# Attention, gated unit and convolution unit on one core: residual added within PSUM, key exponentials behind the x evictions, first output products in pieces

## What is computed

```python
q_s = exp(q - max(q, -1));  q_s = q_s / (sum(q_s, -1) + 1e-9)      # over 64 channels of a head
k_s = exp(k - max(k, 2));   k_s = k_s / (sum(k_s, 2) + 1e-9)       # over the 576 tokens
kv = einsum('bhsd,bhse->bhde', k_s, v)
x = einsum('bhsd,bhde->bhse', q_s, kv)       # (8, 576, 512) after reordering
# first unit
h = gelu_tanh(x @ w_in)                      # 1024 wide: u, v = halves of 512
v_n = layer_norm(v) * g_ln
v_s = einsum('ts,bsd->btd', w_sg, v_n) + b_sg
x1 = x + (u * v_s) @ w_out                   # the residual
# second unit
h = relu(x1 @ w_in2)                         # 1024 wide
c = conv over tokens, 3 taps per channel
y = (h * sigmoid(c)) @ w_out2
```

## Time and profile before

| | us |
|---|---|
| median of 3 runs | 989.21 (989.05 to 991.13) |
| the profiled execution | 990.6 |
| its span, first to last instruction | 988.8 |
| mean granted share of TensorE's clock | 0.988 |

### The profile page before, as it was taken

How to read it: one execution, slowest core, us unless ns; L and a number is a source line. 1 busy time by engine, 2 the same in 40 slices (tenths; PEclk the granted TensorE clock), 3 DMA queues, 4 the chain that set the end, 5 groups by cost and what they waited for, 6 DMA issues and landing times.

```text
span 988.8 us, 15996 instructions
## 1 busy us (share of the span) xinstructions
PE 941.2 (95%) x6652; PEld 909.6 (92%) x6652; DVE 619.8 (63%) x935; ACT 376.7 (38%) x560; POOL 353.1 (36%) x222
## 2 busy tenths in 40 slices
PE   6689899899998998999999998999999999999998
PEld 5589799798897997998998997999999999999998
DVE  6794666656747656667356597676767575757560
ACT  4462442433424424334214344343434343434331
POOL 4642634345436345363303322222222222222230
PEclk8899999999999999999999998999999999999999
DMA  9706115034052151241211421010202011110101
GB/s 312 258 15 193 51 45 176 36 81 167 20 154 92 28 181 49 49 136 35 81 49 43 141 73 61 25 66 19 73 25 74 25 57 41 33 65 13 37 25 48
DMA packets 49911, 77.92 MB, mean 79 GB/s; under 512 B 4272, under 2 KB 22704, under 8 KB 48944
## 3 DMA queue, kind: packets, MB, share of 16 engines
q1 hardware_dynamic: 45232, 67.48, 21.4%
q10 hardware_dynamic: 4608, 9.44, 2.5%
HBM read 56.97 MB, written 18.89 MB: 77 GB/s over the span
## 4 chain that ended last, share of the span: by engine, by line
PE 79%; DVE 9%; issue 5%; ACT 3%; DMA 2%; POOL 1%; ACTq 0%; SPq 0%; POOLq 0%; DVEq 0%
PE psum L417 64%; PE psum L409 6%; PE psum L475 4%; DVE plain_arena L1167 2%; PE psum L451 2%; DVE plain_arena L1164 2%; PE psum L556 2%; PE psum L510 1%; DMA plain_arena<-in_q 1%; ACT split_arena L742 1%; POOL plain_arena L1401 1%; DVE split_arena L1089 1%; ACT plain_arena L769 0%; ACT split_arena L723 0%; POOL split_arena L1395 0%
## 5 line engine op out<-in xcount | busy, mean ns | idle before, releaser
L417 PE MATMUL psum<-split_arena 128*128 128x288 f32 x5568 | 765.9, 298 | 28.3 <-DVE split_arena L1089 16.3
L417 PEld LDWEIGHTS psum<-split_arena 128*128 128x128 f32 x5568 | 750.8, 190 | 36.6 <-DVE split_arena L1089 20.8
L1444 POOL TENSOR_TENSOR plain_arena<-plain_arena 128x576 f32<-128x576 f32 x64 | 107.5, 1680 | 294.7 <-ACT plain_arena L934 294.7
L1307 DVE TENSOR_SCALAR plain_arena<-plain_arena 128x576 f32<-128x576 f32 x64 | 39.8, 622 | 113.8 <-ACT plain_arena L928 113.8
L409 PE MATMUL psum<-split_arena 128*128 128x512 f32 x384 | 96.5, 398 | 4.3 <-DVE plain_arena L1164 2.3
L1312 DVE SCALAR_TENSOR_TENSOR plain_arena<-plain_arena 128x576 f32<-128x576 f32 x64 | 97.0, 1516 | 2.2
L1401 POOL TENSOR_TENSOR plain_arena<-plain_arena 128x576 f32<-128x576 f32 x32 | 47.4, 1482 | 126.8 <-DVE plain_arena L1147 126.8
L409 PEld LDWEIGHTS psum<-split_arena 128*128 128x128 f32 x384 | 70.6, 190 | 20.9 <-DVE plain_arena L1164 4.9
L928 ACT ACTIVATE plain_arena<-psum 128x576 f32<-128x576 f32 x64 | 41.5, 649 | 93.8 <-PE psum L417 59.3
L934 ACT ACTIVATE plain_arena<-plain_arena 128x576 f32<-128x576 f32 x64 | 43.7, 683 | 51.5 <-DVE split_arena L1317 44.7
L1317 DVE TENSOR_TENSOR split_arena<-plain_arena,split_arena 128x576 fp32r<-128x576 f32 x64 | 54.0, 843 | 12.2 <-ACT split_arena L940 11.1
(11 more groups left out here) (79 smaller groups left out, 772.7 us busy)
## 6 DMA issues: line engine op xcount, KB each, us to landing
x_dram<-plain_arena ACTq DMA_DIRECT2D x32, 288.0 KB, 2.1
plain_arena<-x_dram SPq DMA_DIRECT2D x8, 1152.0 KB, 5.5
outT<-plain_arena SPq DMA_DIRECT2D x32, 288.0 KB, 2.1
plain_arena<-in_v SPq DMA_DIRECT2D x32, 256.0 KB, 3.2
plain_arena<-in_kT SPq DMA_DIRECT2D x7, 1152.0 KB, 10.2
plain_arena<-in_k SPq DMA_DIRECT2D x7, 1024.0 KB, 5.7
plain_arena<-in_q SPq DMA_DIRECT2D x7, 1024.0 KB, 5.6
plain_arena<-in_w_in SPq DMA_DIRECT2D x8, 512.0 KB, 5.5
```

What stands on the lines that cost most here:

```text
L417: mm = e.matmul(out[:, h, 0:NH], stat[s], mov[m][:, h * NH:(h + 1) * NH], start=first and n == 0, stop=last and n == 2, skip_group_check=True)
L1444: e.tensor_tensor(gt[:, f % 2, :], gt[:, f % 2, :], hp[:, f % 2, 1:T + 1], ALU.mult).then_inc(hg_full, 1)
```

## The change

- `add_x`: L1164 writes its sum back into the PSUM banks, and the second add reads it there and writes `x1`. All waits of TensorE for `o_half` become waits for `o_add`.
- ScalarE, end of a body: `exp_k(n, 0)` moves behind `hi_x(a, 0)`, `exp_k(n, 1)` behind `hi_x(a, 1)`, `exp_k(n, 2)` behind the last store.
- `kv_piece(b, 0)` waits for `v_tail_sum` in place of `v_gelu`.
- Second half: the first two output tiles of batch 0 are made in pieces, `first_y(f)`, each of the twelve products that need tile f. They stand between the last `h_unit` of batch 0 and around the first of batch 1. ScalarE and VectorE split the x of batch 1 two tiles later, and ScalarE's order of copies follows.

```diff
--- before.py
+++ after.py
@@ -466,11 +466,11 @@
                 else:
                     e.wait_ge(v_in[j % 2], 32 * b + 16 * (j // 2))
                 if j == 0 and not (isinstance(b, int) and b <= 1):
-                    e.wait_ge(o_half, (b - 1) * DT - 1)
+                    e.wait_ge(o_add, (b - 1) * DT - 1)
                 elif j == 0 and b == 1:
                     e.wait_ge(kv_lo, 2)
                 if j == 0 and not first(b):
-                    e.wait_ge(v_gelu, b * NU)
+                    e.wait_ge(v_tail_sum, b)
                 for d in range(DT):
                     mm = e.matmul(kv_sums[:, d // 2, d % 2, 0:VW], kn[:, j, d * P:(d + 1) * P], v_place(b, j)[:, d, :],
                                   start=j == 0 and d % 2 == 0, stop=j == NJ - 1, skip_group_check=True)
@@ -492,11 +492,11 @@
                     e.wait_ge(x_lo, 2)
                 if ds[0] == 0 and not (isinstance(b, int) and b == 0):
                     if u == 0:
-                        e.wait_ge(o_half, b * DT - 3)
+                        e.wait_ge(o_add, b * DT - 3)
                     elif u == 1:
-                        e.wait_ge(o_half, b * DT)
+                        e.wait_ge(o_add, b * DT)
                     else:
-                        e.wait_ge(o_half, b * DT - 1)
+                        e.wait_ge(o_add, b * DT - 1)
                 for d in ds:
                     if u == 0:
                         e.wait_ge(x_lo, b * DT + d + 1)
@@ -574,7 +574,7 @@
                     elif isinstance(b, int) and b == B - 1:
                         e.wait_ge(x_lo, B * DT)
                     else:
-                        e.wait_ge(o_half, b * DT + 2)
+                        e.wait_ge(o_add, b * DT + 2)
                 for f in fs:
                     if d == 0:
                         e.wait_ge(g_lo, b * FT + f + 1)
@@ -654,7 +654,7 @@
 
             def h_unit(b, f):
                 if isinstance(b, int) and b == 0 and f < 2:
-                    e.wait_ge(o_half, B * DT - 3 + f)
+                    e.wait_ge(o_add, B * DT - 3 + f)
                 else:
                     e.wait_ge(h_relu, b * F2T + f - 1)
                 for d in range(DT):
@@ -666,22 +666,25 @@
                                      [x2[h][:, d, :] for h in (0, 1)], d == 0, d == DT - 1)
                 mm.then_inc(h_done, 1)
 
-            def y_unit(b, par, d):
-                if isinstance(b, int) and b == 0:
-                    if d == 0:
+            def y_part(b, par, d, fs):
+                if fs[0] == 0:
+                    if b == 0 and d == 0:
                         e.wait_ge(w2_lo, len(W2))
-                    if d == 0:
-                        e.wait_ge(o_half, B * DT - 1)
-                    elif d == 1:
-                        e.wait_ge(o_half, B * DT)
-                if d >= 2 or not (isinstance(b, int) and b == 0):
-                    e.wait_ge(y_copied, b * DT + d - 1)
-                for f in range(F2T):
+                        e.wait_ge(o_add, B * DT - 1)
+                    elif b == 0 and d == 1:
+                        e.wait_ge(o_add, B * DT)
+                    else:
+                        e.wait_ge(y_copied, b * DT + d - 1)
+                for f in fs:
                     if d == 0:
                         e.wait_ge(hg_lo, b * F2T + f + 1)
                     mm = both_halves(y_sets[d % 2], [w2out[h][:, f, d * P:(d + 1) * P] for h in (0, 1)],
                                      [hg[par][h][:, f, :] for h in (0, 1)], f == 0, f == F2T - 1)
-                mm.then_inc(y_done, 1)
+                if fs[-1] == F2T - 1:
+                    mm.then_inc(y_done, 1)
+
+            def y_unit(b, par, d):
+                y_part(b, par, d, list(range(F2T)))
 
             def step(b, par, last=False):
 
@@ -691,9 +694,27 @@
                         h_unit(b + 1, 2 * d + 1)
                     y_unit(b, par, d)
 
-            for f in range(F2T):
+            def first_y(f):
+                y_part(0, 0, 0, [f])
+                y_part(0, 0, 1, [f])
+
+            for f in range(F2T - 1):
                 h_unit(0, f)
-            step(0, 0)
+                if f >= 4:
+                    first_y(f - 4)
+            h_unit(0, F2T - 1)
+            first_y(3)
+            first_y(4)
+            first_y(5)
+            h_unit(1, 0)
+            for f in range(6, F2T):
+                first_y(f)
+            for f in range(1, 4):
+                h_unit(1, f)
+            y_unit(0, 0, 2)
+            for f in range(4, F2T):
+                h_unit(1, f)
+            y_unit(0, 0, 3)
             step(1, 1)
             for k in range(1, B // 2 - 1):
                 step(2 * k, 0)
@@ -904,12 +925,13 @@
                 for d in range(DT):
                     if a is not None and d >= 2:
                         hi_x(a, d - 2)
+                        if n is not None:
+                            exp_k(n, d - 2)
                     store_x1(m, d)
-                    if n is not None and d >= 1:
-                        exp_k(n, d - 1)
                     if a is None and d == 1:
                         hi_x2(0)
                 if n is not None:
+                    exp_k(n, 2)
                     exp_q(n, 2)
 
             first_attention()
@@ -975,18 +997,21 @@
             e.wait_ge(o_done, B * DT)
             e.wait_ge(o_add, B * DT)
             for f in range(F2T + 2):
-                if f == F2T - 2:
-
-
-                    relu(0, f)
-                    sigmoid(0, f - 1)
+                tile_steps(0, 0, f)
+                if f == F2T - 1:
                     hi_x2(1)
-                    hi_hg(0, 0, f - 2)
-                else:
-                    tile_steps(0, 0, f)
                 if f == 2:
                     hi_w2(len(W2) - 1)
-            step(0, 0)
+            copy_y(0, 0)
+            copy_y(0, 1)
+            for f in range(4):
+                tile_steps(1, 1, f)
+            copy_y(0, 2)
+            for f in range(4, F2T + 2):
+                if f == F2T - 1:
+                    hi_x2(2)
+                tile_steps(1, 1, f)
+            copy_y(0, 3)
             step(1, 1)
             for k in range(1, B // 2 - 1):
                 step(2 * k, 0)
@@ -1160,11 +1185,12 @@
                     e.wait_ge(x1_out[d % 2], b * 32 + 16)
                 elif not (isinstance(b, int) and b == 0):
                     e.wait_ge(x1_out[d % 2], b * 32)
-                place = x1[:, d % 2, :]
-                e.tensor_tensor(place.rearrange("p (a b) -> p a b", a=2), o_set(b, d)[:, :, 0:NH],
-                                f32(xT[0][:, d, :]).rearrange("p (a b) -> p a b", a=2), ALU.add).then_inc(o_half, 1)
+                bank = o_set(b, d)[:, :, 0:NH]
+                e.tensor_tensor(bank, bank, f32(xT[0][:, d, :]).rearrange("p (a b) -> p a b", a=2),
+                                ALU.add).then_inc(o_half, 1)
                 e.wait_ge(o_half, b * DT + d + 1)
-                e.tensor_tensor(place, place, f32(xT[1][:, d, :]), ALU.add).then_inc(o_add, 1)
+                e.tensor_tensor(x1[:, d % 2, :].rearrange("p (a b) -> p a b", a=2), bank,
+                                f32(xT[1][:, d, :]).rearrange("p (a b) -> p a b", a=2), ALU.add).then_inc(o_add, 1)
 
             def lo_x2(b):
                 for d in range(DT):
@@ -1322,7 +1348,7 @@
                 for f in range(F2T + 2):
 
 
-                    if x and f == (F2T - 2 if isinstance(b, int) and b == 0 else F2T - 1):
+                    if x and f == (F2T if b == 0 else F2T - 1):
                         lo_x2(b + 1)
                     if f < F2T:
                         convolve(b, f)
```

## The result

| | us |
|---|---|
| before, on the same chip | 989.13 (988.53 to 991.13, 4 runs) |
| after | 973.24 (972.04 to 973.87, 4 runs) |
| ratio | 0.9834, 95% interval 0.9817 to 0.9852 |
| profiled execution of after | 973.65, its span 971.9 |

The account below looks back on a forecast made before the run. TensorE, busy 941 of 988.8 us, was taken to bound the kernel, so only its idle stretches counted. 14.6 − 0.8 + 2.5 − 0.8 = 15.5 us off gave a median of 973.7, range 969.5 to 979.5.

Parts of the forecast that it names:

- boundaries m = 0 to 5: Between batches, `x_piece(a, 2)` starts at 312.20 instead of 314.63: 2.43 us gained, six times, 14.6 us.
- new wait at m = 6: At the last boundary nothing is gained and TensorE waits for tile 1's second add: 0.8 us lost.
- key product's wait, six times: `kv_piece(a, 0)` waiting for `v_tail_sum` gains 0.42 us for m = 1 to 6: 2.5 us.
- second half: Stops of 4.0 and 1.4 us replace the 4.9 one, and the clock falls again: 0.8 us lost.
- The held add: Tile 1's second residual add at a boundary, 2.17 us beside GpSimd's `sub_k`, takes 0.76 when reading PSUM.
- The rival in which it stays held: The second add takes 2.17 us whether reading PSUM or not: 982.3 us, chance 0.08.
- the slower rival: The add writing into PSUM is itself held by GpSimd's three `sub_k`: 1008.7 us, chance 0.05.
- The new wait: At a boundary TensorE stands 0.72 us before `o_part(m, 3)`, until tile 1's second add frees the bank.
- What is next late: At a boundary `v_part` 1 wants tile 3 at 310.43 and starts at 310.83: fits by 0.4 us.
- the restart after a stop: The first product of TensorE after a stop costs 0.1 us more.
- late pieces: Rival: second-half pieces find their inputs late and cost some 3 us beyond the sum: 976.5 us, chance 0.10.
- the case with the clock at 2.4 GHz: Rival: TensorE's clock doesn't fall in the second half, 2.5 us less: 971.2 us, chance 0.25.

Follow-up runs that it names:

- the first run: The kernel before with only the residual adds going through PSUM and TensorE's waits moved to the second add: 978.40 us, ratio 0.9891.
- the bank exchange: The changed kernel with the two main PSUM bank pairs exchanged between output tiles 0 and 1 of the first unit: 971.39 us, ratio 0.9809.
- the later run without the stop: The changed kernel with the first six pieces waiting for only the first seven weight chunks, the eighth awaited ahead of the seventh piece: 966.58 us, ratio 0.9770.

## Why the prediction was right

The forecast of 973.7 lay 0.5 from the median. In the profile, which the sum was made from, it lay further off: a span of 973.3 was forecast and 971.9 measured, so the sum was 1.4 short. That the median hides most of this is luck, since the profiled execution of before was one of the slower ones (990.6 against 989.13). The pieces of the sum are these:

| step of the prediction | forecast | measured |
|---|---|---|
| boundaries m = 0 to 5 | 14.6 | 6 × 2.55 = 15.3 |
| new wait at m = 6 | −0.8 | −0.81 |
| key product's wait, six times | 2.5 | 6 × 0.52 = 3.1 |
| first half, up to `h_unit(0, 0)` | 16.3 | 17.7 (568.29 − 550.57) |
| second half | −0.8 | −0.8 |

- **The held add.** The value was taken from the add at 303.75, which had a PSUM input. It was right: all 32 are between 757 and 759 ns. The rival in which it stays held is out by this, the slower rival by the first adds (L1189), which write PSUM beside `sub_k` in 0.76 too (all 32 between 755 and 767 ns), as expected from L1077.
- **The new wait.** It was forecast at 0.72 and 0.1 for the restart, and 0.81 more than before was lost, seven times. The mechanism is right: the first run shows it with the residual alone, the bank exchange shows it gone. That the size fits so closely is partly luck. The whole stop costs 0.98, and 0.18 of that was lost in the kernel before already, since TensorE came to `o_part(m, 3)` at about 304.48, just ahead of the release at 304.50, and not behind it at 304.63 as the prediction had it.
- **What is next late.** The prediction named tile 3 for `v_part` 1 with 0.4 of room. In the changed kernel it fits, as forecast. With the new wait taken away `v_part` 1 stands idle for 0.17.
- **A term too small:** the restart after a stop, 0.1, was counted for the new stop but not for those that go at `x_piece(a, 2)` and `kv_piece`; each removed stop gave 0.08 to 0.11 at its second product, beyond what its first product gained. That is 0.2 of the 0.22 per batch that the sum was short.
- **Not in the sum:** 0.4 gained in start-up and 0.2 lost just before the second half. Both lie beside what the change touches: the stop in the first body that waits for `lo_x` was between 2.0 and 4.2 in the profiles of these kernels.
- **The second half.** Both stops came as worked out, 3.95 and 1.30 against 4.0 and 1.4, and the clock fell again, for 2.3 against 2.5. In the range of the forecast the case with the clock at 2.4 GHz was a fourth of the chance; the profile shows the low stretch, and the later run without the stop shows none. Whether the clock falls in every execution isn't shown (see the four times of the kernel with the bank pairs exchanged). The Trainium skill (TensorE: Matmul & The Clock Gate, "What's actually happening") ties the low clock to idleness before it, and the run without the stop agrees: 1.00 from 565 to 583.

- **The range.** Its upper end was explained as late pieces and half of the held add's loss. From the prediction's own numbers that would be 973.7 + 2.8 + 4.3 = 980.8, and not 979.5. Nothing else hangs on it.

The span fell by 1.0 more than the medians. A profile is one execution, and start-up alone moves it by as much: the first residual add starts between 99.4 and 101.7 in the profiles of these kernels.

## What to carry to other kernels

Find what TensorE waits for last at the stop, and follow the chain back until an instruction is longer than its twins; what held it here was on an engine that isn't in the chain at all. Two edits on one chain need not add (here 2.0 and 1.58 alone, 2.56 together): cost them together, in one schedule of the stretch, and name what is late next and by how much. A piece of work that is moved forward to fill a gap moves its waits forward too, and a wait that was free at its old place (here for a weight chunk that the piece doesn't even read) can become the stop.

## Of the hardware, not expected

- GpSimd was held by VectorE as well as the other way round. `sub_k` on 128x1024 took 2.90 us with the adds from SBUF beside it, also with ScalarE's order changed alone (2.91), and 2.38 in the changed kernel and in that with the residual in PSUM alone, though nothing of it was edited. The Trainium skill (SBUF — State Buffer, "SBUF: two separate sides") has it that whichever starts first holds the other for the whole instruction; the rows agree in kind: the first `sub_k` starts at 303.17, inside an add from SBUF that runs from 303.07 to 303.83, and takes 0.5 longer. It was not on the path here.
- At full clock TensorE loses 0.08 to 0.11 us beyond each stop: the second product after it comes that much late (309.68 to 310.58 for six, where six take 0.80).
